# Attention and two mixtures of experts on one core: the combination and G made per batch, G in column tiles and spread by transfers

## What is computed

```python
def mab(q, kv):                       # C = 128, scale = 1/sqrt(C)
    s = scale * (q @ kv.transpose(0, 2, 1))
    a = exp(s - s.max(-1)); a /= a.sum(-1) + 1e-09
    return a @ kv
h = mab(I, x)                         # x: 2 x 11456 x 128, I: 32 inducing points
y = mab(x, h)                         # 2 x 11456 x 128
# moe: expert by argmax of cos(x, expert_emb) / tau, gate by softmax
out[mask] = gate[mask] * (relu(x[mask] @ w1[e]) @ w2[e])   # E = 8, F = 1024
# moe2: expert by argmax of x @ w_gate + modality_bias[modality_id]; the same form, other weights
```

## Time and profile before

| | |
|---|---|
| time, median of 3 runs | 1071.93 us (1071.9 to 1072.4) |
| the profiled execution, its own time | 1073.95 us |
| its span | 1072.2 us |
| busy: TensorE, VectorE, ScalarE, GpSimd | 92%, 71%, 63%, 19% |
| mean granted TensorE clock | 0.959 |
| transfers | 70.99 MB |

### The profile page before, as it was taken

The page is one execution under the profiler, slowest core; times in us unless marked ns, Lnnn a source line. Parts: engine busy times, 40 slices in busy tenths (PEclk is TensorE's granted clock), DMA queues, the critical chain, the costliest instruction groups (busy, mean ns, idle before and its releaser), DMA issues.

```text
span 1072.2 us, 27216 instructions
## 1 busy us (share of the span) xinstructions
PE 986.6 (92%) x6367; PEld 498.5 (46%) x6367; DVE 763.1 (71%) x2221; ACT 679.6 (63%) x1622; POOL 205.1 (19%) x437
## 2 busy tenths in 40 slices
PE   7766845899999999999999999999999999999887
PEld 5544322345444444444445444454444444444443
DVE  4676765667778777787777778677787777877654
ACT  4654544466666666666766666666666666667554
POOL 6870011111111111111111111111111111111100
PEclk9786886899999999999999999999999999999999
DMA  8995431010110101111010110101101011110000
GB/s 334 417 350 192 147 105 32 19 48 24 40 33 24 48 24 43 30 29 43 24 48 25 38 35 24 48 24 39 33 24 48 24 43 30 29 43 24 17 23 21
DMA packets 52216, 70.99 MB, mean 66 GB/s; under 512 B 33326, under 2 KB 39254, under 8 KB 50889
## 3 DMA queue, kind: packets, MB, share of 16 engines
q1 hardware_dynamic: 52169, 70.41, 20.6%
HBM read 40.81 MB, written 23.55 MB: 60 GB/s over the span
## 4 chain that ended last, share of the span: by engine, by line
PE 85%; DVE 4%; DMA 3%; issue 3%; ACT 3%; POOL 1%; ACTq 0%; SPq 0%; DVEq 0%; POOLq 0%
PE y L1298 44%; PE up L1321 23%; PE up L1311 7%; PE y L1375 2%; PE TB L1337 1%; PE TB L1361 1%; PE SM L1349 1%; PE up L1237 1%; DMA GW<-in_x 1%; ACT W1B L552 1%; DMA W1B<-in_moe_w 1%; DMA wraw<-in_moe_w 1%; PE SM L1369 1%; DVE GW L729 1%; DVE W1B L735 1%
## 5 line engine op out<-in xcount | busy, mean ns | idle before, releaser
L881 DVE SCALAR_TENSOR_TENSOR hlo<-up,hhi 128x500 f16<-128x500 f32 x736 | 493.7, 671 | 167.2 <-ACT hhi L607 164.3
L607 ACT ACTIVATE hhi<-up 128x500 f16<-128x500 f32 x736 | 424.2, 583 | 166.7 <-PE up L1321 81.3
L1321 PE MATMUL up<-ytb,W1B 128*128 (+1 forms) x1104 | 274.3, 378 | 10.3 <-issue 10.0
L1298 PE MATMUL y<-hhi,W2A 128*128 128x500 f16 x736 | 218.0, 378 | 10.4 <-DVE hlo L881 5.5
L1298 PE MATMUL y<-hhi,GW 128*128 128x500 f16 x736 | 215.6, 374 | 0.4 <-DVE hlo L881 0.4
L1321 PEld LDWEIGHTS up<-ytb,W1B 128*128 x1104 | 108.1, 98 | 145.5 <-issue 35.4
L1311 PE MATMUL up<-E4T,GW 128*128 (+1 forms) x368 | 138.9, 380 | 0.0
L1298 PE MATMUL y<-hlo,W2A 128*128 128x500 f16 x368 | 138.5, 376 | 0.0
L1298 PE MATMUL y<-hlo,GW 128*128 128x500 f16 x368 | 137.4, 373 | 0.0
L1298 PEld LDWEIGHTS y<-hhi,W2A 128*128 x736 | 68.0, 97 | 92.5 <-issue 45.3
L516 POOL TENSOR_TENSOR st<-ss,root 125x4 f32<-125x4 f32 x46 | 46.9, 1019 | 246.1 <-ACT TB L633 246.1
(11 more groups left out here) (164 smaller groups left out, 1043.3 us busy)
## 6 DMA issues: line engine op xcount, KB each, us to landing
wraw<-in_moe_w SPq DMA_DIRECT2D x24, 512.0 KB, 4.9
xth<-x_turned SPq DMA_DIRECT2D x46, 250.0 KB, 2.8
out<-yout SPq DMA_DIRECT2D x46, 250.0 KB
GW<-in_x SPq DMA_DIRECT2D x10, 1024.0 KB, 8.8
x_turned<-GW SPq DMA_DIRECT2D x10, 1000.0 KB, 10.3
W1B<-in_moe_w SPq DMA_DIRECT2D x8, 512.0 KB, 11.0
x_turned<-GW SPq DMA_DIRECT2D x2, 750.0 KB, 7.1
GW<-in_x SPq DMA_DIRECT2D x1, 768.0 KB, 12.9
```

The source lines that it names most:

```text
L607: nc.scalar.activation(hhi[:, (u % UP) * CT:(u % UP + 1) * CT], ups[u % UP][:, 0:CT], ACT.Relu).then_inc(s["hi_done"], 1)
L881: nc.vector.scalar_tensor_tensor(hlo[:, o:o + CT], ups[u % UP][:, 0:CT], 0.0, hhi[:, o:o + CT], ALU.max, ALU.subtract).then_inc(s["lo_done ...
L1298: ins = mm(y[:, 0:CT], W[:, bass.ds(woff + (fb * 2 * C + o), C)], h[:, k * CT:(k + 1) * CT], start=opens and fb == 0 and n == 0, stop=fb = ...
L1321: ins = mm(ups[k][:, 0:CT], W1B[:, bass.ds(woff + (wl * F + fb * P), P)], ytb[:, bass.ds(yoff + yl * CW, CT)], start=n == 0, stop=n == 2)
```

## The change

1. **Combination per batch.** The functions `turn_max`, `max_back`, `join`, `turn_h`, `spread_h` (TensorE), `spread_max`, `negate_max`, `weigh`, `scale_points`, `split_points`, `low_h4` (VectorE) and `shares`, `high_h4` (ScalarE) do it for one batch b. For batch 0 they stand in quads 6 (`CHAIN_AT`) to 8 of the pooling; for batch 1 around steps -4 and -3.
2. **G per batch, column-tiled.** One bank holds four pieces of 32 rows (an expert's half each), each from a matmul with the 32 columns of `HT` as weights. Eight banks take the place of 32. ScalarE and VectorE make each bank's two halves (`tmp16`), SP stores them to `g_split` and loads them back twice, as the 128 rows that E4T needs. Batch 0's banks are made in quads 9 and 10, batch 1's in steps -2 and -1 and behind them. W1A is loaded once for each batch, at quads 4 to 7 and at pooling's end.
3. **W2B** gets a slot for each expert (`raw_slot`) and is split around the filling steps: 0 to 2 before step -3, 3 and 7 before -2, 4 to 6 before -1.
4. **Buffers.** Quad slot 0 lies in `early`, which later holds E4T and `ytb`; `hhi`, `hlo`, `yT`, `yout` lie in `wst`. W1B has three slots instead of four.
5. **Loop.** Step 0 is written out on every engine; the loop runs over 1 to 41 (`steps_from_1`).
6. **Small.** The expert constants move from quads 6 and 8 to 3 and 5; the router multiplies by 1/tau and takes one reciprocal for gates and sums together, two VectorE instructions fewer.

The diff, cut to its core (SP's part, then `high_g` and the steps of ScalarE, `low_g` of VectorE, `g_product` and the steps of TensorE):

```diff
+                if 0 <= q - W1A_AT < 4:
+                    load_w1a(0, 2 * (q - W1A_AT))
+                    load_w1a(0, 2 * (q - W1A_AT) + 1)
+                if q == CHAIN_AT + 4:
+                    store_g(0, 0)
+                    store_g(0, 1)
+                    for e in range(4):
+                        load_w2b(e)
+                if q == CHAIN_AT + 5:
+                    store_g(0, 2)
+                    store_g(0, 3)
...
+            def load_g(b):
+                for k in range(2):
+                    sp.wait_ge(s[f"g_stored{k}"], 64 * (b + 1))
+                for k in range(2):
+                    sp.dma_start(G[k * 2 * M:(k + 1) * 2 * M, b * GB:(b + 1) * GB],
+                                 GD[b].rearrange("h m n -> (h m) n")).then_inc(s[f"g_loaded{b}"], 16)
...
             sp_step(-4)
+            load_g(0)
+            for e in (7, 4, 5, 6):
+                load_w2b(e)
+            sp.wait_ge(s["mixed_in"], NQ - 1)
+            for e in range(4):
+                load_w1a(1, e)
+            sp.wait_ge(s["w_lo_ready"], NE)
+            for e in range(4, 7):
+                load_w1a(1, e)
+            sp_step(-3)
+            sp.wait_ge(s["w2b_lo_ready"], 5)
+            load_w1a(1, 7)
             sp.sem_inc(s["out_free"], 1)
-            for c in range(-3, NCH):
+            sp_step(-2)
+            store_g(1, 0)
+            sp_step(-1)
+            store_g(1, 1)
+            store_g(1, 2)
+            sp_step(0)
+            store_g(1, 3)
+            load_g(1)
+            for c in range(1, NCH):
                 sp_step(c)
...
+            def high_g(b, k):
+                n = b * 4 + k
+                act.wait_ge(s["g_product"], n + 1)
+                if n >= 2:
+                    act.wait_ge(s[f"g_stored{n % 2}"], 32 * (n // 2))
+                nc.scalar.activation(tmp16[:, n % 2, 0, :], gbank(b)[:, :], ACT.Copy).then_inc(s["g_hi_ready"], 1)
...
+            shares(1)
+            act_step(-4)
+            act.wait_ge(s["mixed_in"], NQ)
+            for slot in range(XT_N):
+                act.wait_ge(s[f"x_stored{slot}"], 16 * len(range(slot, NQ, XT_N)))
+            for e in (0, 1, 2):
+                high_down(e)
+            act_step(-3)
+            high_h4(1)
+            for e in (3, 7):
+                high_down(e)
+            act.wait_ge(s["w2b_lo_ready"], 5)
+            act_step(-2)
+            high_g(1, 1)
+            for e in LATE_W2B:
+                high_down(e)
+            act_step(-1)
+            high_g(1, 3)
+            act_step(0)
+            steps_from_1(act, act_step)
...
+            def low_g(b, k):
+                n = b * 4 + k
+                v.wait_ge(s["g_hi_ready"], n + 1)
+                nc.vector.tensor_tensor(tmp16[:, n % 2, 1, :], gbank(b)[:, :], tmp16[:, n % 2, 0, :],
+                                        ALU.subtract).then_inc(s["g_lo_ready"], 1)
...
+            def g_product(b, k):
+                n = b * 4 + k
+                for e in (2 * k, 2 * k + 1):
+                    pe.wait_ge(s[f"w1a_loaded{b}{e}"], 16)
+                if k >= 1:
+                    pe.wait_ge(s["g_lo_ready"], n)
...
+                for i in range(4):
+                    units = w1a_slot(b, 2 * k + i // 2).rearrange("p (c f) -> p f c", f=NF)
+                    ins = mm(gbank(b)[i * M:(i + 1) * M, :].rearrange("p (f c) -> p f c", c=P), HT[:, b * M:(b + 1) * M],
+                             units[:, i % 2 * 4:i % 2 * 4 + 4, :], start=True, stop=True)
+                ins.then_inc(s["g_product"], 1)
...
-            all_steps(pe, pe_step)
+            pe.wait_ge(s["ht16_ready"], 2)
+            pe_step(-4)
+            join(1)
+            turn_h(1)
+            pe.wait_ge(s["h4_ready"], 1)
+            pe_step(-3)
+            spread_h(1)
+            pe.wait_ge(s["g_loaded0"], 32)
+            pe.wait_ge(s["w2a_steps"], 3 * NE)
+            pe.wait_ge(s["h4_ready"], NB)
+            pe_step(-2)
+            g_product(1, 1)
+            pe_step(-1)
+            g_product(1, 3)
+            pe.wait_ge(s["w_lo_ready"], NE)
+            pe.wait_ge(s["w2b_lo_ready"], NE)
+            pe.wait_ge(s["g_lo_ready"], 4 * NB)
+            pe_step(0)
+            pe.wait_ge(s["g_loaded1"], 32)
+            pe.wait_ge(s["ht16_ready"], 2 * NB)
+            steps_from_1(pe, pe_step)
```

460 lines of the change are left out of this document (280 added, 180 removed).

## The result

| | before | changed |
|---|---|---|
| time, median (range, runs) | 1072.16 us (1071.9 to 1075.1, 4) | 1101.07 us (1099.9 to 1106.3, 4) |
| ratio to before, 95% interval | | 1.0273 (1.0251 to 1.0295) |
| span of the profiled execution | 1072.2 us | 1098.1 us |

What follows compares the result with a forecast made beforehand. TensorE bounds the main part from 197 us; only the stages ahead can move, with pooling held by ScalarE and VectorE in turn. -26.5 + 5.5 + 6.2 + 3.1 + 3.0 = -8.7: 1065.2 us profiled, 1063 median, range 1049 to 1074.

Steps and rivals of the forecast that it cites:

- Step 0 is written out ... +3.0 (bounds 0 and 3.2): Step 0 to step 1: one more entry into new code on TensorE, an issue idle of +3.0 us.
- What is late next is SP's queue ... 20.8 us, to 125.4: Before step -3: first E4 transpose waits behind 7.9 MB of loads at 380 GB/s; first matmul at 127, -26.5 us.
- rival B: SP's queue: the transposed tile does not wait behind the 7.9 MB; 11.2 us less, 1052 us; chance 0.12.
- Step -3 to -2, +5.5: Filling steps: `spread_h`, its high half, W2B splits and hops add 5.8 us, a shorter router takes 0.3 off.
- -2 to -1, +6.2: Filling steps: a G product behind the units, its high half, W2B splits and hops +6.5, router -0.3 us.
- Step -1 to 0, +3.1: Last filling step: two G products at 0.94 us each and an eviction with hops +3.4, router -0.3 us.
- Pooling, +6.1: Quads 6 to 10: batch 0's combination and G put between ScalarE and VectorE; last exponential at 105.3 instead of 99.24.
- Batch 1's G at 0: During step 0: storing and loading 2.1 MB, some 5 us plus 3 of waiting, fits before step 1; cost 0.
- Rival D: Filling steps -3 to -1: they hide their new work; 14.8 us less, 1048 us; chance 0.08.
- rival E: Filling steps: they hide nothing and hand-overs cost about half again, +8 us; 1071 us, no change; chance 0.12.
- rival F: G's banks: column tiles do not run side by side, 3.76 us a bank, +22.6; 1086 us; chance 0.03.
- Rival C: Pooling turns transfer-bound, 15.1 us of W1A and W2B loads uncovered; 1078 us; chance 0.10.

Runs made afterwards that it cites:

- run 12: Run 9's kernel with G's product reading runs of four neighbouring float32 and writing its bank permuted: median 1064.16 us, ratio 0.9926 to the kernel before.
- run 8: Changed kernel with step 0 back in the loop on all engines, the wait for batch 1's G at each loop step's end: 1083.94 us.
- run 9: Changed kernel with run 2's SP order and step 0 back in the loop on every engine: 1069.2 us.
- run 2: Changed kernel, SP issuing step -3's transpose ahead of the G, W2B and W1A loads, and batch 1's W1A loads behind step -2's transpose too: 1079.41 us.
- run 5: Kernel before with, on TensorE alone, a copy of step 0 ahead of the loop that a branch always skips: 1088.88 us.
- run 7: Kernel before with 290 skipped matmuls on TensorE ahead of the loop: 1082.26 us.
- run 10: Changed kernel with G's products reading 512 neighbouring columns of W1A instead of every eighth: 1096.04 us.
- run 11: Changed kernel with batch 0's W1A loads cut to 32 of 128 rows and its products summing over these alone: 1100.21 us.

## Why the prediction was wrong

Most of its structure was right, but one mechanism was missing and two sizes were wrong. Missing was that a written-out step moves all code behind it; mis-sized were the first transpose's wait in SP's queue and the time of a bank of G. With all three undone (run 12) the kernel takes 1064.16 us where the changed one takes 1101.07, so together they are worth 36.9 us, and this rests on several executions at both ends. Undone one after another they give 17.1 (run 8), 14.7 (run 9 against 8) and 5.0 (run 12 against 9). These add up to 36.9 because each run is subtracted from the one before it; that is no test of the parts, each of which is from single executions. The parts also depend on the order: with SP's order undone first, it gives 21.7 (run 2) and the written-out step 10.2 (run 9 against 2). Counted in the traces from step 0's layer 2 to the end, the written-out step is worth 15.1 us in one pair and 13.4 in the other. That run 12 lands near the forecast of 1063 confirms nothing: the forecast was for a kernel whose step -3 starts at 127, behind 20.8 us of queue, and run 12's starts at 117.7 without it.

- *What bounds the kernel*: right. The loop changed by 1.6 us in 781, and everything else is ahead of or behind it.
- *"Step 0 is written out ... +3.0 (bounds 0 and 3.2)"*: this step failed furthest beyond its bounds, and here the mechanism was wrong too. The forecast counted one more entry into new code. That local cost came: from step 0 to step 1 it took 2.0 us more. But the term as a whole measured 13 to 17 us in the changed kernel, because TensorE's code behind step 0 was moved, and every entry there changed: behind the loop the gaps of 2.79, 3.18, 0 and 0.93 us became 3.02, 2.58 with 2.59, 2.72 and 3.78. Behind the exit that is 7.6 us more of idle; longer groups of matmuls, next point, make up about the rest of the 11.0. The upper bound was the error: the rows of before showed that such gaps exist and differ (3.18 and none in neighbouring steps of like code), and a cost that differs by place without a known reason has no bound from one place. The rule of "Runtime: NRT & Kernel Launch", Instruction fetch mechanics, in the Trainium skill (code is fetched ahead in blocks of 256 instructions, and a taken branch out of the window stalls) is compatible with runs 5, 7 and 8 and was the warning to take in earnest. The prediction took from it one more gap of known size and not that all later code changes its place. That the gaps are fetches of code was not shown; that moving the code lengthens the end by some 10 us was, in both kernels.
- *Twelve matmuls behind a gap*: a part of the loss is beside the idle. In the changed kernel the first group behind the loop takes 4.08 us, with a granted clock of 0.65, where such a group takes 2.70 in the loop, and the stretch behind it has 1.00:
```profile
1014.57:1018.65 4.08, 4.08 (x13) 1.61 (x14) 2.00 (x4) 1.76 (x3) 0.00 (x0) 0.65 0.04 6
1019.00:1030.00 11.00, 10.89 (x72) 5.17 (x71) 8.95 (x30) 7.27 (x21) 2.09 (x6) 1.00 0.01 1
```
  A share of 1.00 is 2.4 GHz, 0.50 is 1.2. So a gap of some 3 us can cost 1.4 us again, but not always: the groups behind gaps of 3.18 (before) and 2.72 (changed) take 2.70. This first group was already slow before (4.00). New are the 0.80 with 3.91 us from 1037.19 on and the 4.35 at 1078.88, where the kernel before has 2.70 each: from the exit on, the four groups take 3.8 us more in all. The forecast left this out.
- *"What is late next is SP's queue ... 20.8 us, to 125.4"*: the mechanism was right (the transpose waited for the loads, rival B falls), the size was not. 11.4 us were lost ahead of the first load (pooling 4.2 more, a wait for stores of 5.3, and what SP issues between), and the 7.9 MB took 27.7 us to the first matmul instead of 22.4, since the first part ran at 187 GB/s. The worse of the bounds (landed at 132) was passed by 11.5. What I had priced from loads of 128 rows were now stores and loads of other shapes: the 2.1 MB of G alone take some 12 us, by batch 1's loads, where the sum had 5.5, and these 6 us are about the 5.3 that the queue was over.
- *Step -3 to -2, +5.5, and -2 to -1, +6.2*: measured 6.1 and 6.2. The first is right. The second has some luck in it: its product behind the units took 2.02 us instead of 0.94, and with the faster read the stretch is 0.7 us shorter (20.0 in run 10, 20.1 in run 12), so the other parts were a little too high.
- *Step -1 to 0, +3.1*: measured 8.9. The two products took 2.04 and 2.02 us where I had 0.94 each, and the gap ahead of layer 2 is 5.53 instead of 3.09. With the faster read the stretch is 2.7 us shorter (run 10; 2.8 in run 12 against 9). With the 2.4 of the gap, these are 5.1 of the 5.8 us beyond the forecast. Why the gap is longer was not tried.
- *Pooling, +6.1*: measured 10.2. One cause was tested, the other only read. The 0.94 us of a bank came from products that read 512 float32 in one run; the changed product reads one in eight, as the diff's `rearrange` says, and I priced it by its columns alone. In quad 9 runs 10 and 12 give 0.9 us of this back; by the last exponential run 10 gives 1.9, which the scatter covers. The 2.9 in quads 3 to 5 is put down to GpSimd from VectorE's rows beside GpSimd's alone. No run took it away, and 2.9 us is itself less than the scatter of pooling, so its cause stays open.
- *Batch 1's G at 0*: right, with less room than forecast: loading took some 12 us and not 5, and was over at 221, some 10 us ahead of step 1's layer 2.
- *Rival D* (nothing costs in the filling steps), *rival E* (8 us more in the hand-overs) and *rival F* (tiles in turn) don't describe what came. Rival C (transfer-bound pooling) fell with run 11. None of the rivals had the code's place as a mechanism, and beside the size of SP's queue (12.5 us from pooling's end to step -3) that was the largest error.

## What to carry to other kernels

Writing out a step of a loop was not free on an engine whose program has branches: compare the idle time put down to issue at each entry, at every stage behind the edit too, and measure the edit alone. When a stage is filled with early loads, list what the one latency-bound transfer on that queue stands behind, for each of the next steps, since moving only the first such transfer ahead moves the wait to the second. A product that is cheap by its columns should be checked for the stride of what it reads before it is put between instructions that work in turn.

## What was not expected of the hardware

- A copy of 581 instructions that is never executed made the kernel 14.5 us slower when it stood ahead of the loop on TensorE, and 4.5 (near the scatter of single executions) at the end of the program. Behind the loop, far from the copy, the end was 10.9 us longer, and the single gaps there are not proportional to the copy's length.
- Four column tiles that read float32 at a stride of 32 bytes take 2.02 us for 4 times 512 columns; with runs of 16 bytes, or one run of 2 KB, 1.03 to 1.07. The number of rows (32 or 128) makes no difference.
- A VectorE instruction of 128x8 took 1.86 us, and one of 128x128 took 2.05 instead of 0.29, beside GpSimd's work.
- Two loads of G, 64 rows of 16 KB each, take some 12 us for 2.1 MB with nothing beside them, at 221 GB/s and a share of 1.05. Weight loads of 128 rows reach 377 GB/s at 1.00. What in the loads of G makes them slow was not tried.
